# Attention, gated product and routed experts in one kernel: the router's steps, the row buffers and the weight loads in another order

## The reference

```python
# 1: attention in chunks of 32 queries; each sees 16 keys to the left, its own 32, 8 to the right, and 8 memory keys
scores = scale * np.matmul(q_c, k_full.transpose(0, 1, 3, 2))
a = np.exp(scores - max); a = a / (sum + 1e-9)
out[:, :, c_start:c_end] = np.matmul(a, v_full)
# 2: a gated product, w_in [512, 2048], w_out [2048, 512]
h = x @ w_in
x = (h * np.cos(h)) @ w_out
# 3: eight experts; a token passes by when x @ w_skip <= 0
e_idx = np.argmax(xc @ w_gate, axis=1)       # xc: the tokens that don't
h = np.maximum(xc[mask] @ w1[e], 0.0)        # w1 [8, 512, 1024]
y[mask] = gate_w[mask, None] * (h @ w2[e])   # w2 [8, 1024, 512]
out[do_compute] = xc + y
```

## Time and profile before

| what | value |
|---|---|
| median of 3 runs | 874.37 us (872.95 to 878.34) |
| profiled execution | 874.06 us |
| its span, first to last instruction | 872.4 us |
| PE busy | 822.0 us (94%) |
| DVE busy | 511.7 us (59%) |
| ACT busy | 465.6 us (53%) |
| POOL busy | 81.3 us (9%) |
| mean granted TensorE clock | 0.983 |
| instruction fetch | 67 packets of the queue q8 |

### The profile page before, as it was taken

One profiled execution on the slowest core, in us unless ns is written; L12 is line 12 of the kernel. 1 busy time (PEld: TensorE's weight loads), 2 busy tenths in 40 slices (PEclk: granted clock), 3 DMA queues, 4 the chain that ended last, 5 costly groups with the idle time before them and its releaser, 6 DMA issues. The chain is left out here.

```text
span 872.4 us, 19559 instructions
## 1 busy us (share of the span) xinstructions
PE 822.0 (94%) x8088; PEld 726.4 (83%) x8089; DVE 511.7 (59%) x1045; ACT 465.6 (53%) x819; POOL 81.3 (9%) x108
## 2 busy tenths in 40 slices
PE   5799999999999999999999999999998799999994
PEld 3688888888888888888888888888987688999993
DVE  4577655565565556556565555565545568766651
ACT  3477755555555556555655655554544455554430
POOL 2000000010001000000100010010301512111100
PEclk9799999999999999999999999999999889999997
DMA  9822031104211310311031122002009837555300
GB/s 334 308 87 69 25 110 62 62 25 134 62 62 45 128 62 26 109 62 62 26 134 62 62 75 97 26 1 74 13 32 375 318 132 269 204 203 204 125 14 25
DMA packets 40027, 93.82 MB, mean 108 GB/s; under 512 B 6559, under 2 KB 6559, under 8 KB 39936
## 3 DMA queue, kind: packets, MB, share of 16 engines
q1 hardware_dynamic: 35968, 86.01, 28.2%
q0 software_dynamic: 3968, 6.52, 2.3%
HBM read 78.16 MB, written 17.00 MB: 109 GB/s over the span
## 5 line engine op out<-in xcount | busy, mean ns | idle before, releaser
L845 PE MATMUL h_ps<-xT_hi,in_hi 128*128 128x384 f32 x512 | 180.3, 352 | 1.4 <-DVE xT_lo L1228 1.4
L845 PE MATMUL h_ps<-xT_hi,in_lo 128*128 128x384 f32 x512 | 172.7, 337 | 0.0
L845 PE MATMUL h_ps<-xT_lo,in_hi 128*128 128x384 f32 x512 | 172.4, 337 | 0.0
L859 PE MATMUL y_ps<-out_hi,g_hi 128*128 128x512 f32 x384 | 151.6, 395 | 5.6 <-DVE g_lo L1333 5.6
L859 PE MATMUL y_ps<-out_hi,g_lo 128*128 128x512 f32 x384 | 152.4, 397 | 0.0
L859 PE MATMUL y_ps<-out_lo,g_hi 128*128 128x512 f32 x384 | 151.9, 395 | 0.0
L1045 ACT ACTIVATE hs<-h_ps 128x384 f32<-128x384 f32 x128 | 62.5, 488 | 163.9 <-PE h_ps L845 162.9
L1327 DVE TENSOR_SCALAR whole<-us 128x384 f32<-128x384 f32 x128 | 45.1, 352 | 134.4 <-ACT us L1046 134.0
L1069 ACT ACTIVATE us<-us 128x384 f32<-128x384 f32 x128 | 67.2, 525 | 75.3 <-DVE us L1329 74.9
L845 PEld LDWEIGHTS h_ps<-xT_hi,in_hi 128*128 128x128 f32 x512 | 96.8, 189 | 4.7 <-DVE xT_lo L1228 1.8
L845 PEld LDWEIGHTS h_ps<-xT_lo,in_hi 128*128 128x128 f32 x512 | 96.8, 189 | 1.7
(11 more groups left out here) (179 smaller groups left out, 1281.8 us busy)
## 6 DMA issues: line engine op xcount, KB each, us to landing
raw_a<-w SPq DMA_DIRECT2D x32, 512.0 KB, 6.9
raw_b<-w SPq DMA_DIRECT2D x32, 512.0 KB, 7.1
k_sb<-qk SPq DMA_DIRECT2D x22, 512.0 KB, 4.5
v_sb<-v SPq DMA_DIRECT2D x22, 512.0 KB, 3.6
x_mid<-x SPq DMA_DIRECT2D x24, 256.0 KB, 4.7
out<-x SPq DMA_DIRECT2D x24, 256.0 KB, 5.2
q_sb<-qk SPq DMA_DIRECT2D x22, 256.0 KB, 3.0
in_raw<-w_in SPq DMA_DIRECT2D x4, 1024.0 KB, 11.2
```

What stands on the lines that cost most here:

```text
L845: last = pe.matmul(h_ps[:, f % 2, 0:BN], w[:, dc, f * P:(f + 1) * P], x[:, half, dc, :], start=(n == 0), stop=(n == 3 * DC - 1))
L859: last = pe.matmul(y_ps[:, j, :], g[:, f % RING, j * P:(j + 1) * P], w[:, f, :], start=(f == 0 and n == 0), stop=(f == FT - 1 and n == 2))
```

## The change

- The router's steps of a block stand at other sites: logits of the third tile 27 to 23, `route` 28 to 24, `rexp` 29 to 25, `gate` 30 to 26, `ranks` 30 to 27, `place` 31 to 28. After the last block, `gate` comes ahead of `place`.
- SP issues in1 and out0 after the second `values` (`v_full` 2) and no longer after the second scores, then q, k and v of tile 3, then in2 and out1 after the first `up` (`h_full` 1), in3 and out2 after the third, out3 after the fourth.
- There are three buffers for gathered rows (`xg_a`, `xg_b`, `xg_c`), slot s uses number s % 3, and slot s gathers for s + 2. After the last block the lists of slots 1, 0 and 2 are loaded, then the rows of 1, 0 and 2 gathered, and only then the other five lists loaded.
- SP's loads of the second half of slot 1's weights wait for slot 1's gather.
- PE turns the rows of slot 1 in the middle of `half(0, 0)`, DVE does `rows_low(1)` ahead of `finish(0, 0)`.
- The further slots are no loop but eleven bodies, each nested in the condition of the one before.

```diff
-ROUTER = [(5, "x1", 0), (7, "logits", 0), (11, "x1", 1), (15, "logits", 1), (19, "x1", 2), (27, "logits", 2),
-          (28, "route", 0), (29, "rexp", 0), (30, "gate", 0), (30, "ranks", 0), (31, "place", 0)]
+ROUTER = [(5, "x1", 0), (7, "logits", 0), (11, "x1", 1), (15, "logits", 1), (19, "x1", 2), (23, "logits", 2),
+          (24, "route", 0), (25, "rexp", 0), (26, "gate", 0), (27, "ranks", 0), (28, "place", 0)]
...
-        xg = [xg_a, sb("xg_b", [P, 2, D])]
+        xg = [xg_a, sb("xg_b", [P, 2, D]), sb("xg_c", [P, 2, D])]
...
-            with eng.Fori(E // 2, NSLOT // 2) as r:
-                with eng.If(2 * r < used):
-                    run(2 * r, 0)
-                with eng.If(2 * r + 1 < used):
-                    run(2 * r + 1, 1)
+            with ExitStack() as nest:
+                for s in range(E, NSLOT - 1):
+                    nest.enter_context(eng.If(s < used))
+                    run(s, s % 2)
...
-        def rows_landed(s, par):
-
-            return 16 * (s + 2 - par) + (32 if par == 0 else 0)
+        def rows_buffer(s):
+
+            return s % 3
+
+        def rows_landed(s):
+
+            return 32 * (s // 3 + 1) + (32 if s % 3 == 0 else 0)
...
-            sp.wait_ge(s_full, 2)
+            sp.wait_ge(v_full, 2)
             load_in(1)
             load_out(0)
-
-            sp.wait_ge(v_full, 1)
             load_qk(3, flat(q_sb), flat(k_sb), qk_ld)
             load_v(3, flat(v_sb), v_ld)
-            sp.wait_ge(v_full, 3)
-            for n in range(2, 4):
-                load_in(n)
-                load_out(n - 1)
+            sp.wait_ge(h_full, 1)
+            load_in(2)
+            load_out(1)
+            sp.wait_ge(h_full, 3)
+            load_in(3)
+            load_out(2)
+            sp.wait_ge(h_full, 4)
             load_out(3)
...
                 wait(sp, w2lo_done, 4 * (s - 1))
+                if isinstance(s, int) and s == 1:
+                    sp.wait_ge(xg_ld[1], rows_landed(1))
...
             pool.wait_ge(xg_ld[0], 32)
             carry(pool)
-            for s in (1, 0):
+            for s in (1, 0, 2):
                 load_list(s, s * N, list_ld[s])
-            for s in range(2, E):
-                load_list(s, s * N, lists_ld)
             for n in range(BT):
                 pool.wait_ge(x1_st[n], 32 * BLOCKS)
-            pool.wait_ge(ready, 9)
+            pool.wait_ge(ready, 10)
             pool.wait_ge(list_ld[1], 16)
             carry(pool)
-            gather(1, 1, 1)
+            gather(1, 1)
 
             pool.wait_ge(list_ld[0], 32)
             pool.wait_ge(xg_full, 2)
             carry(pool)
-            gather(0, 0, 0)
-            pool.wait_ge(lists_ld, 16 * (E - 2))
+            gather(0, 0)
+            pool.wait_ge(list_ld[2], 16)
+            carry(pool)
+            gather(2, 2)
+            for s in range(3, E):
+                load_list(s, s * N, lists_ld)
+            pool.wait_ge(lists_ld, 16 * (E - 3))
 
             def run_slot(s, par):
-                if 1 <= s < E - 1:
+                if 1 <= s < E - 2:
                     pool.wait_ge(o_done, 2 * s)
                     carry(pool)
-                    gather(s + 1, 1 - par, s + 1)
+                    gather(s + 2, s + 2)
                 scatter(s, s)
...
                 for f in range(EFT):
+                    if s == 0 and a == 0 and f == EFT // 2:
+                        turn_rows(1)
...
             def run_slot(s, par):
                 up_slot(s)
                 if 1 <= s < E - 1:
-                    turn_rows(s + 1, 1 - par)
+                    turn_rows(s + 1)
                 wait(pe, o_done, 2 * s - 1)
                 half(s, 0)
-                if s == 0:
-                    turn_rows(1, 1)
                 second_half(s)
...
             route(BLOCKS, "route", 0)
+            route(BLOCKS, "gate", 0)
             route(BLOCKS, "place", 0)
-            route(BLOCKS, "gate", 0)
...
                     tables()
-                finish(s, par, 0, s)
                 if s == 0:
                     rows_low(1)
+                finish(s, par, 0, s)
                 finish(s, par, 1, s)
```

More of the change, by code:

```diff
@@ L300, in program @@
         emptied = sem("emptied")
-        list_ld = [sem(f"list_ld{n}") for n in range(2)]
+        list_ld = [sem(f"list_ld{n}") for n in range(3)]
         lists_ld = sem("lists_ld")
@@ L305, in program @@
         table_done = sem("table_done")
-        xg_ld = [sem(f"xg_ld{n}") for n in range(2)]
+        xg_ld = [sem(f"xg_ld{n}") for n in range(3)]
         scattered = [sem(f"scattered{n}") for n in range(2)]
@@ L616, in load_list, with gather @@
                                ).then_inc(landed, 16)
-            def gather(s, par, where, stored=N):
+            def gather(s, where, stored=N):
+                to = rows_buffer(s)
                 for a in range(2):
                     pool.indirect_dma_start(
-                        out=xg[par][:, a, :], out_offset=None, in_=x_mid[0:stored, :],
+                        out=xg[to][:, a, :], out_offset=None, in_=x_mid[0:stored, :],
                         in_offset=bass.IndirectOffsetOnAxis(ap=listed[:, where, a, 0:1].bitcast(I32), axis=0),
-                        bounds_check=stored - 1, oob_is_err=False).then_inc(xg_ld[par], 16)
+                        bounds_check=stored - 1, oob_is_err=False).then_inc(xg_ld[to], 16)
             def scatter(s, where):
@@ L649, in _ @@
             carry(pool)
-            gather(0, 0, 0, N - BN)
+            gather(0, 0, N - BN)
             pool.wait_ge(h_full, BLOCKS * FT)
@@ L655, in _ @@
             pool.memset(xg[1][:, :, :].rearrange("p a d -> p (a d)"), 0.0).then_inc(ready, 1)
+            pool.memset(xg[2][:, :, :].rearrange("p a d -> p (a d)"), 0.0).then_inc(ready, 1)
             sort(BLOCKS - 1)
@@ L693, in run_more @@
                 carry(pool)
-                gather(s, par, E)
+                gather(s, E)
                 scatter(s, E)
@@ L929, in _, with turn_rows @@
                 last.then_inc(xg_full, 1)
-            def turn_rows(s, par):
-                pe.wait_ge(xg_ld[par], rows_landed(s, par))
+            def turn_rows(s):
+                pe.wait_ge(xg_ld[rows_buffer(s)], rows_landed(s))
                 for a, bank in enumerate((turn[:, 0, :], s_ps[:, 0, :])):
@@ L937, in turn_rows @@
                     for dc in range(DC):
-                        last = pe.transpose(bank[:, dc * P:(dc + 1) * P], xg[par][:, a, dc * P:(dc + 1) * P], ident[:, :])
+                        last = pe.transpose(bank[:, dc * P:(dc + 1) * P], xg[rows_buffer(s)][:, a, dc * P:(dc + 1) * P], ident[:, :])
                     last.then_inc(xg_full, 1)
@@ L983, in run_slot @@
                 if 1 <= s < E - 1:
-                    turn_rows(s + 1, 1 - par)
+                    turn_rows(s + 1)
                 wait(pe, o_done, 2 * s - 1)
                 half(s, 0)
-                if s == 0:
-                    turn_rows(1, 1)
                 second_half(s)
             def run_more(s, par):
-                turn_rows(s, par)
+                turn_rows(s)
                 up_slot(s)
@@ L1249, in route @@
                     last_one = isinstance(B, int) and B == BLOCKS
-                    k = [{"route": 0, "gate": CHOSEN + (6 if last_one else 1), "place": CHOSEN + (1 if last_one else 4)}[step]]
+                    k = [{"route": 0, "gate": CHOSEN + 1, "place": CHOSEN + 4}[step]]
                     bc = [P, BT, E]
@@ L1266, in route @@
                         then(dve.reciprocal(pairs[:, :, 1:2], gate_sum[:, :].unsqueeze(2)))
-                        assert k[0] == (ROUTE if last_one else CHOSEN + 4)
+                        assert k[0] == CHOSEN + 4
                         return
@@ L1281, in route @@
                         then(dve.tensor_tensor(filled_to[:, :], filled_to[:, :], turn[:, 0, BT * E:(BT + 1) * E], ALU.add))
-                        assert k[0] == (CHOSEN + 6 if last_one else ROUTE)
+                        assert k[0] == ROUTE
                         if not last_one:
@@ L1452, in finish @@
                 if isinstance(s, int) and s == 0:
-                    dve.wait_ge(xg_ld[0], rows_landed(0, 0))
+                    dve.wait_ge(xg_ld[0], rows_landed(0))
                 carry(dve)
-                dve.scalar_tensor_tensor(o_sb[:, a, :], y_ps[:, a, :], listed[:, where, a, 1:2], xg[par][:, a, :],
+                dve.scalar_tensor_tensor(o_sb[:, a, :], y_ps[:, a, :], listed[:, where, a, 1:2], xg[rows_buffer(s)][:, a, :],
                                          ALU.mult, ALU.add).then_inc(o_done, 1)
```

## The result

The changed kernel takes **859.8 us** (median, 859.1 to 860.1) against 874.7 (873.0 to 878.3) for the kernel before on the same chip (four runs of each; the 874.37 of the table was the median of the first three): ratio 0.9831, 95% interval 0.9813 to 0.9849. The profiled execution took 860.12 us with a span of 858.5. The forecast was 858.5 us (854.5 to 864.5): inside its range, 1.3 us too low.

What follows compares the result with a forecast made beforehand. TensorE, busy 822.0 of 872.4 us, was taken as the bound, so only its idle or lower-clock time could be won. Terms 2.6 + 2.0 + 7.25 + 1.5 + 1.0 + 1.2 = 15.55 off 874.06 gave 858.5 us, range 854.5 to 864.5.

Steps and rivals of the forecast that it cites:

- part 1: Middle blocks: moved router sites end the wait at the ranks, with a new 0.57 us wait for `route`; 2.6 us gained.
- part 2: Prologue: later weight loads remove the 1.95 us instruction stop in the third values step; 2.0 us gained.
- part 3: Slots: slot 1 starts 7.25 us earlier, higher clock gives 1.5, no gather wait at slot 3 gives 1.0.
- part 4: End: one far jump replaces POOL's rounds over the further slots; 1.2 us gained.
- the term put at nothing: Last block: the third buffer's memset (0.9 us) lies under POOL's wait and costs nothing.
- holding back the 2 MB: Before slot 1: rings without these weights let scatters land at about 675 and slot 1's rows at about 685.
- The other zero of the last block: Last block: `gate` ahead of `place` costs nothing since DVE stands idle for the ranks; 0.6 us otherwise.
- (a): Prologue rival: the instruction stop stays, the packet being late by its own nature and not by load; 860.5 us, chance 0.13.
- (b): Prologue rival: the clock stays up, 1.6 us more gained; 856.9 us, chance 0.10.
- (c): Slot 1 rival: the gather is no earlier and PE stops inside `half(0, 0)`; 864.0 us, chance 0.08.
- (d): Middle blocks rival: two ACT table visits and `route` delay PE, each block waiting 4.26 us; 880.4 us, chance 0.03.
- (e): Prologue and end rival: later loads and nested form give nothing; 861.7 us, chance 0.06.

Runs made afterwards that it cites:

- s2_logits21: The changed kernel with the third tile's logits at site 21 and `route` at 23, `rexp` 25, `gate` 26: 856.9 us.
- s1_route25: The changed kernel with `route` at site 25, `rexp` at 26 and `gate` at 27: 857.8 us.
- x_first: The changed kernel with `w_in` step 1 behind the third values step in the prologue, so DVE does `x_sb` ahead of `in_lo`: 858.8 us.
- the last kernel: The changed kernel with logits at site 21 and `route` at 23, `xg_b` and `xg_c` memsets behind the last sort, `x_sb` ahead of `in_lo`: 853.4 us.
- u_hold: The changed kernel without the wait of the second half of slot 1's weights for slot 1's gather: 860.0 us.
- p2_loads: The kernel before with only the later marks for SyncE's weight loads: 872.5 us, ratio 0.9984.

## Why the prediction was right, point by point

The sum was 1.6 us too large against the profiled pair (15.55 forecast, 13.94 measured). By terms, forecast less measured: part 1 0.7, part 2 0.2, part 3 -0.2, part 4 0.1, the term put at nothing 0.9, the rest -0.1.

**Part 1, 2.6 us forecast, 1.91 measured.** The mechanism was right: no wait at the ranks, a new one from `route` ahead of `sum`. The wait is 0.17 us as a gap and 0.33 in the distance of starts (2.52 from the `up` at 248.82 to 251.34, 2.19 without a wait), smaller than the forecast 0.57. But the `down` itself starts where the prediction put it: at 253.43 in the clock of the kernel before, which is 251.32 here, since the `up` of f = 11 starts 2.11 us earlier (241.55 before, 239.44 now); measured 251.34. PE came 0.26 us later than forecast, at 251.01 in place of 250.75. The third tile's logits had stood in one place with `values` and now stand alone: the `down` ahead of them takes 2.18 us and not 2.08 to the next start, the `up` behind 2.21 (244.18 to 246.39) and not 2.11. These 0.2 us are no loss as long as DVE is later than PE; they only shorten the wait. `s2_logits21` has no such wait, and there sharing a place was worth 0.2 us a block (553.37 against 554.47 us in `s1_route25`, over six blocks).

What made the term too large stands behind that `down`. The wait before was 0.97 (3.14 from 260.47 to 263.61 in the earlier trace rows, 2.17 without a wait), not 1.05. The ranks take 0.31 us where they took 0.23. And the `down` behind the new wait takes 2.21 where it took 2.17. With smaller differences either way the distance from block to block fell by 0.31 (79.25 to 78.94), where 0.44 was forecast.

**Part 2, 2.0 forecast, 1.94 to the first `up`, 1.82 at the end of block 0.** The stop went for the stated reason: no weights lie ahead of the packet. That the size came out was in part luck. Half of the stop was cover for another wait, the one for `x_sb`, which DVE does behind `in_lo` (1.91 in place of 0.88), so 0.92 us are left of the 1.95. The rest the prediction had left out or put at nothing: the third values step is 0.37 shorter (1.23 in two pieces before, 0.86 in one), the transposes at the higher clock take 0.46 less to the first `up` (2.50 and 2.04), and the values step began 0.20 earlier. And the clock in block 0 differs between executions. From the first `up` to the second `down` that waits it is 25.9 us in those that keep the clock near 37 us, 26.5 to 27.4 in those with a second fall there, and 24.0 in the two (`x_first` and the last kernel) where it does not fall at the first `up` either. So this term has over a microsecond of noise.

**Part 3, 7.25 + 1.5 + 1.0 forecast, 7.30 + 1.42 + 1.23 measured.** Right in size. Late next was DVE, as said: it ends `rows_low(1)`, and slot 1 starts, with no wait on a gather before it. Of its reasons one carries no time: holding back the 2 MB (`u_hold`). Three lists ahead and the early turn are enough, as far as these runs tell; neither was tried alone. The close match owes something to the execution: in the kernels that keep the old slots' order the distance from slot 0 to slot 1 is 24.97 to 26.92 us.

**A term put at nothing that cost 0.89 us.** "The third buffer's memset lies under POOL's wait for the last block: nothing." It does lie under POOL's wait, but beside the last fraction on DVE, and DVE stood still for it. This step failed; it is the largest error in the sum (0.9 of 1.6 us), with part 1's 0.7 next. The other zero of the last block held: with `gate` ahead of `place` the stretch from the last wait to slot 0 is 18.87 us, 18.91 before.

**Part 4, 1.2 forecast, 1.10 measured** (1.28 with the nested form alone). POOL's jump took 2.9 us, as forecast, and the prediction's own working gives 1.1. PE's jump took 4.0 us, not 2.9, and is hidden behind POOL.

**The rivals.** (a) is refuted by `p2_loads`; (b) did not happen in the profiled execution but does in `x_first` and in the last kernel: to the first `down` that waits it is worth 1.4 us (8.83 from the first `up`, 10.21 in the changed kernel), near its 1.6, and 1.5 more come from the second fall, which it did not name; (c) and (d) did not happen; (e) is refuted for both parts.

## What to carry to other kernels

When a step is moved, count what it leaves behind and where it now stands alone: sharing a place between two large products was worth 0.2 us a block here, once no wait of PE hid it. The whole move of the router's steps won 0.3. An idle engine is no free place: GpSimd's memset cost DVE, and DVE cost PE, nearly its whole length, and a few operations later it cost nothing. Where a stop is removed, look for the wait that stood behind it, since it takes over part of the gain.

## What the runs showed of the hardware that was not expected

- A DVE operation of 0.36 us took 1.30 us beside two memsets of GpSimd on other data, though the second started 0.14 us after it (648.62 and 648.48).
- The instruction packet's arrival followed the volume in the other queue: 17.0 to 18.5, 18.5 to 19.0 and 20.0 to 21.0 us with 0, 1 and 2 MB issued ahead of it, and with 2 MB it came while the rings were full (DMA share 1.11).
- A place with a small product between two large ones costs PE about 0.1 us on either side besides its own length.
- The granted clock in block 0 differs between executions of near-equal code: with a wait of 2.29 us before the first `down` it stayed at 1.00 in two, with 1.90 to 2.27 it fell to 0.50 in others. The two are also the only ones where it had not fallen at the first `up`, and both do `x_sb` ahead of `in_lo`. After 2.20 us of waiting before slot 1 the windows show 0.58 and 0.57, after 1.14 to 1.67 they show 1.00. What decides in block 0 stays open.
